# A linear-attention and expert kernel: shorter load queue, small zero matmuls, tiles amid the turns

## The chip, the cores and the metric

The kernel runs on one core of a Trainium2 chip. The metric is the time of one execution on the device in microseconds (us): lower is better. TensorE (PE) multiplies, VectorE (DVE), ScalarE (ACT) and GpSimd (POOL) do elementwise work, SyncE (SP) issues the loads and stores, and 16 DMA engines carry them. The engines run side by side and wait for each other through semaphores.

## The reference

Three steps follow one another. First a decayed linear attention without softmax, then a mixture of four ReLU experts, then a feed-forward layer with the Mish function. Everything is float32.

```
# q, k, v: 2 batches, 8 heads, 576 positions, 64 per head
scores = q @ k^T / sqrt(64)
x = (scores * gamma_h ** (i - j) for j <= i, else 0) @ v      # -> 1152 tokens x 512
p = domain_probs / (domain_probs.sum(-1) + 1e-9)              # 1152 x 4
y = sum over e of p[:, e] * (relu(x @ w1[e]) @ w2[e])         # w1: 4 x 512 x 1024
out = mish(y @ w_in) @ w_out                                  # 512 -> 2048 -> 512
```

## The kernel before

**Attention.** The 576 positions are cut into nine places of 64. Place c (the prediction calls its data pair c) needs two loads of 512 KB: `feats` (k and q by features) and `toks` (v and k by tokens). Four buffers (`SLOTS`) hold them, so place c shares a buffer with place c - 4. The loop over turns runs c = 0 to 8 on PE. In turn c PE first does `scores_and_state(c)`: the scores of place c + 1 (L442) and the update of the running state with place c (L447), interleaved; then `output(c)`: `of_state` (L470), which applies the state before place c, and `of_chunk` (L474), which applies the masked scores of place c. Each `pe.matmul` of float32 shows as two records with two weight loads, so `scores_and_state` is 64 records, and each half of `output` is 32.

The other engines serve this loop, each in a written order: POOL's `v_decay(c + 2)` (L1024) decays v of a place once its `toks` has landed; DVE's `masked(c)` (L812) masks the scores, `decayed(c - 1)` (L829) takes the output out of PSUM, `first_lo` (L836) and ACT's `first_hi` (L692) split it into a high and a low part; ACT's `state_copy(c)` (L686) copies the state for the next place. `rows(i)` (L818) makes tables of decay on DVE.

**Tiles amid the attention.** The first 384 of the 1152 tokens are complete after turn 2 (place 0, 1, 2). With them PE can start the first layer of expert 0: a tile is 12 matmuls of 384 columns (`plain_products`, L494 to L496, the three products of high and low parts). `TILES_IN` lists which of the eight tiles follow `output(c)` in which turn. Each tile needs its weights split: ACT's `job_hi` (L368), then POOL's `job_lo` (L395), listed by turn in `JOBS_IN`. In each turn POOL does `v_decay(c + 2)` first and then the jobs of the turn. `plain_ready` waits for the low part of the tile's weights and for the low parts of x (`s_xl`).

**Loads.** SP issues everything in one written order: the first load, `toks` 0, `feats` and `toks` of places 1 to 3 one after the other, then for each place from 4 on two weight loads of 256 KB (`WEIGHTS_IN`), a wait for `output(c - 4)` to free the buffer, and the pair; then the identity matrix and all other weights.

**Zero matmuls.** `keep_warm` multiplies zeros into bank 7: seven times 512 columns before the first load has landed, and five times after the scores of place 0.

**Behind the attention.** PE does `second(0, ...)`, 12 groups of three matmuls of 512 columns, and then stage 2, where one level of Strassen's scheme is used for the other 768 tokens: its products P1 and P2 use x directly (P1 of stage 2 waits for all nine `first_lo`), P6, P7, P5 and P4 use differences of blocks of x, made by DVE (L959 to L964), split by ACT's `t_hi` (L736) and DVE's `t_lo` (L918). P6 also waits for ACT's copy of P1 (`keep`, L722), which stands on ACT behind the `t_hi` and two weight jobs.

Of the kernel before, what the change touches and what calls it, by code (L numbers as in the profile page):

```python
# [13 lines left out]
P = 128  # L14
# [5 lines left out]
CH = 64  # L20
PLACES = SEQ // CH
PAIRS = HEADS // 2
MID = SEQ // 2
SLOTS = 4
# [8 lines left out]
KT = DM // P  # L33
# [13 lines left out]
def has_state(c):  # L47
# [5 lines left out]
STATE_BANK, OUT_BANK = 2, 3  # L53


TILES_IN = {3: (0,), 4: (1,), 5: (2, 3), 6: (4,), 7: (5, 6), 8: (7,)}
JOBS_IN = {1: (("w1", 0, 0),), 2: (("w1", 0, 1), ("w1", 0, 2)), 3: (("w1", 0, 3),), 4: (("w1", 0, 4), ("w1", 0, 5)),
           5: (("w1", 0, 6),), 6: (("w1", 0, 7), ("w2", 0, 0)), 7: (("w2", 0, 1), ("w2", 0, 2), ("s", 0, 0)),
           8: (("w2", 0, 3), ("w2", 0, 4)), 9: (("w2", 0, 5),)}

WEIGHTS_IN = (2, 2, 2, 2, 2)
ROWS_IN = {4: 5, 5: 6, 6: 7, 7: 8}
PROBS_IN = 5
WARM_START, WARM_NEXT = 7, 5

# [3 lines left out]
ITEMS = 4  # L71
# [98 lines left out]
def build(nc, first_in, feats_in, toks_in, ident_in, probs_in, weights_in, out):  # L170
    with ExitStack() as ctx:
# [125 lines left out]
        def landed(c):  # L297
            return 16 * (c // SLOTS + 1)
# [101 lines left out]
        @block.sync  # L400
        def _(sp):
            def load_feats(c):
                sp.dma_start(slots[:, c % SLOTS, 0:2], feats_in[c - 1]).then_inc(s_feats[c % SLOTS], 16)

            def load_toks(c):
                sp.dma_start(slots[:, c % SLOTS, 2:4], toks_in[c]).then_inc(s_toks[c % SLOTS], 16)

            def load_weights(r):
                job, e, layer, u = LOADS[r]
                if r >= RAW:  # L410
                    sp.wait_ge(s_wl, LOADS[r - RAW][0] + 1)
                sp.dma_start(w_raw[:, r % RAW], weights_in[2 * UNITS * e + UNITS * layer + u])\
                  .then_inc(s_raw[r % RAW], 16)

            sp.dma_start(loaded[:, lead - CONSTS:lead + 2 * KIND], first_in).then_inc(s_feats[0], 16)
            load_toks(0)
            for c in range(1, SLOTS):
                load_feats(c)
                load_toks(c)
            at = 0  # L420
            for c in range(SLOTS, PLACES):
                for r in range(at, at + WEIGHTS_IN[c - SLOTS]):
                    load_weights(r)
                at += WEIGHTS_IN[c - SLOTS]
                sp.wait_ge(s_o, c - SLOTS + 1)
                load_feats(c)
                load_toks(c)
            sp.dma_start(ident[:, :], ident_in).then_inc(s_id, 16)
            for r in range(at, len(LOADS)):
                load_weights(r)  # L430
            by_rows = out.rearrange("(g p) d -> p g d", p=P)
            sp.wait_ge(s_af, read(EXPERTS - 1, TT - 1))
            sp.dma_start(by_rows[:, 0:TT, :], acc_sb[:, 0:TT, :]).then_inc(s_out, 16)
            for g in range(TT, TPP):
                sp.wait_ge(s_af, read(EXPERTS - 1, g))
                sp.dma_start(by_rows[:, g, :], acc_sb[:, g, :]).then_inc(s_out, 16)
            sp.wait_ge(s_out, 16 * (1 + TPP - TT))

        @block.tensor
        def _(pe):  # L440
# [73 lines left out]
            def plain_products(s, i, tiles):  # L514
# [6 lines left out]
                if KT - 1 in tiles:  # L521
                    mm.then_inc(s_l1, 1)

            def product(s, j):

                e, g = s // STAGES, s % STAGES - 2
                n = sums(s)
                if j == P1:
                    if g == 0 and e >= MOE_EXPERTS:
                        pe.wait_ge(s_mi, mish_done(s - 1, 2))  # L530
                    elif g == 0:
                        pe.wait_ge(s_hl, ITEMS * (s - 1) + 3)
                    else:
                        pe.wait_ge(s_cc, ITEMS * (n - 1) + C21 + 1)
                    if s == 2:
                        pe.wait_ge(s_xl, PLACES)
                    if s == MOE_STAGES + 2:
                        pe.wait_ge(s_x2l, SPLIT_AT[2, KT - 1])
                if j == P2:
                    if g == 0 and e >= MOE_EXPERTS:  # L540
                        pe.wait_ge(s_mi, mish_done(s - 1, 3))
                    elif g == 0:
                        pe.wait_ge(s_hl, ITEMS * (s - 1) + 4)
                    else:
                        pe.wait_ge(s_cc, ITEMS * (n - 1) + C12 + 1)
                if j == P6:
                    pe.wait_ge(s_wl, JOB["s", e, g] + 1)
                if j in (P6, P7, P4):
                    pe.wait_ge(s_pt, 3 * n + (P6, P7, P4).index(j) + 1)
                if j in (P5, P3):  # L550
                    pe.wait_ge(s_cc, ITEMS * n + (C11 if j == P5 else C22) + 1)
                if e % MOE_EXPERTS == 0 and g == 0 and X_OF[j][0] == "t":
                    pe.wait_ge(s_tl, 4 * (e > 0) + T_ORDER.index(X_OF[j][1]) + 1)
                for k in range(KH):
                    at = slice(P * k, P * (k + 1))
                    if WEIGHTS_OF[j][0] == "w":
                        row, half = WEIGHTS_OF[j][1:]
                        cs = slice(P * (KH * half + k), P * (KH * half + k + 1))
                        w = w_hi[0][:, 2 * g + row, cs], w_lo[0][:, 2 * g + row, cs]
                    else:  # L560
                        w = w_sum(g)[:, 0, WEIGHTS_OF[j][1], at], w_sum(g)[:, 1, WEIGHTS_OF[j][1], at]
                    i = KH * X_OF[j][1] + k
                    x = (xb_hi[:, i], xb_lo[:, i]) if X_OF[j][0] == "x" else (xt[:, 0, i], xt[:, 1, i])
                    mm = three(banks[BANK_OF[j]][:, 0:TC], w, x, j in OPENS and k == 0, k == KH - 1,
                               skip_group_check=True)
                mm.then_inc(s_l1, 1)
# [49 lines left out]
            def keep_warm(count):  # L616

                for _ in range(count):
                    pe.matmul(banks[7][:, :], zeros[:, 0:P], zeros[:, :], start=True, stop=True)

            pe.wait_ge(s_zt, 1)
            keep_warm(WARM_START)
            pe.wait_ge(s_feats[0], landed(0))
            for h in range(HEADS):
                score(0, 0, h)
                mm = score(0, 1, h)
            mm.then_inc(s_sc, 1)
            keep_warm(WARM_NEXT)
            for c in range(PLACES):
                if has_state(c):  # L630
                    scores_and_state(c)
                output(c)
                for t in TILES_IN.get(c, ()):
                    s, i = divmod(t, ITEMS)
                    plain_ready(s, i)
                    plain_products(s, i, range(KT))

            for q in range(ITEMS * TT):
                second(0, q)
# [38 lines left out]
        def _(act):  # L678
# [53 lines left out]
            def t_hi(e, n):  # L732

                i = T_ORDER[n]
                act.wait_ge(s_tf, (9, 8, 6, 10)[n] if e else (3, 2, 1, 4)[n])
                act.activation(x_sum(i, 0), x_full(e, i), ACT.Copy).then_inc(s_th, 1)  # L736

            for c in range(TURNS):
                if c > 0:
                    first_hi(c - 1)  # L740
                for t in TILES_IN.get(c - 1, ()):
                    plain_hi(*divmod(t, ITEMS))
                if has_state(c):
                    state_copy(c)
                if c == PROBS_IN:
# [5 lines left out]
                for job in IN_TURN.get(c, ()):  # L751
                    if JOBS[job][0] != "s":
                        job_hi(act, job)
            for n in range(4):
                t_hi(0, n)
            for job in IN_STAGE[1]:
                job_hi(act, job)

            for s in range(2, ALL_STAGES):
                e, k = divmod(s, STAGES)  # L760
# [47 lines left out]
        def _(dve):  # L808
# [126 lines left out]
            for c in range(TURNS):  # L935
                if c < PLACES:
                    masked(c)
                if c == 0:
                    for i in range(2, 5):
                        rows(i)  # L940
                if c > 0:
                    decayed(c - 1)
                if c > 1 and c != PER_BLOCK + 1:
                    first_lo(c - 2)
                if c == PER_BLOCK:
                    first_lo(c - 1)
                for t in TILES_IN.get(c - 1, ()):
                    plain_lo(*divmod(t, ITEMS))
                if c in ROWS_IN:
                    rows(ROWS_IN[c])  # L950
                if c == PROBS_IN + 1:
                    probs()
            first_lo(PLACES - 1)


            b11, b21 = xf[:, 0:KH, 0:TC], xf[:, KH:, 0:TC]
            b12, b22 = xf[:, 0:KH, TC:], xf[:, KH:, TC:]
            full = [x_full(0, i) for i in range(4)]
            dve.tensor_tensor(full[0], b12, b11, ALU.subtract).then_inc(s_tf, 1)  # L959
            dve.tensor_tensor(full[2], b22, b12, ALU.subtract).then_inc(s_tf, 1)  # L960
            dve.wait_ge(s_tf, 1)
            dve.tensor_tensor(full[1], b22, full[0], ALU.subtract).then_inc(s_tf, 1)  # L962
            dve.wait_ge(s_tf, 3)
            dve.tensor_tensor(full[3], full[1], b21, ALU.subtract).then_inc(s_tf, 1)  # L964
            dve.wait_ge(s_tf, 4)
            for n in range(4):
                t_lo(0, n)

            for s in range(2, ALL_STAGES):
# [120 lines left out]
```

## Time and profile before

| | before |
|---|---|
| median of three runs | 621.67 us (620.61 to 621.79) |
| the profiled execution's own time | 622.52 us |
| its span | 620.7 us |
| PE busy in the span | 605.9 us, 98% |
| DVE, ACT, POOL busy | 264.0, 234.7, 278.2 us |
| moved by DMA | 50.47 MB |
| mean granted PE clock | 0.989 |

The span is the stretch between the first and the last instruction that the profiler shows; the execution's own time has 1.8 us more around it. Busy time of PE is that of its matmuls, whose ends are modelled. The granted clock is told as a share of full speed: 1.00 is 2.4 GHz, 0.50 is 1.2 GHz. In the lists of waits an idle stretch is put down to what ended it; "issue" means that the profile shows nothing that the engine waited for.

### The profile page before, as it was taken

What the parts mean: (1) busy time and instruction counts of PE and PEld (TensorE: products, weight loads), DVE (VectorE), ACT (ScalarE), POOL (GpSimd) and SP (SyncE); (2) the same over time, 40 slices, a digit from 0 to 9 for tenths busy, and PEclk for the clock granted to TensorE, in tenths of its full rate; (3) what the DMA queues carried; (4) which work ended last, traced back from release to release, by engine and by line L of the source; (5) the groups of instructions that cost most, each with busy time, mean ns of one, the idle gap of its engine ahead of it and who ended that gap; (6) DMA issues with size and microseconds to landing.
All of it is one profiled execution on the core that took longest, in us unless ns stands there. A gap on an engine that the chain in (4) does not pass through costs nothing.

```text
span 620.7 us, 9829 instructions
## 1 busy us (share of the span) xinstructions
PE 605.9 (98%) x4016; PEld 547.0 (88%) x4016; DVE 264.0 (43%) x361; ACT 234.7 (38%) x434; POOL 278.2 (45%) x230
## 2 busy tenths in 40 slices
PE   6799999999999999999999999999999999999997
PEld 4699799999999999999999999989989999989996
DVE  2467654423154434154534154535545432324334
ACT  2464433322323332223432123435455454334431
POOL 2658645535335544435552535532446553443300
PEclk9699999999999999999999999999999999999999
DMA  8963202332112331112322112321211232201002
GB/s 345 331 213 109 80 35 68 104 101 68 35 35 68 103 103 57 46 35 68 102 84 62 58 34 69 102 69 37 67 34 49 69 105 84 68 1 52 1 1 101
DMA packets 24923, 50.47 MB, mean 81 GB/s; under 512 B 2864, under 2 KB 2992, under 8 KB 24880
## 3 DMA queue, kind: packets, MB, share of 16 engines
q1 hardware_dynamic: 24736, 49.84, 25.1%
q8 instruction: 32, 0.52, 0.3%
q14 instruction: 11, 0.09, 0.1%
q10 hardware_dynamic: 144, 0.02, 0.0%
HBM read 47.49 MB, written 2.36 MB: 80 GB/s over the span
## 4 chain that ended last, share of the span: by engine, by line
PE 92%; DVE 2%; ACT 2%; issue 1%; DMA 1%; POOL 1%; SPq 0%
PE bank L494 30%; PE bank L496 29%; PE bank L495 29%; PE bank L442 1%; DMA loaded<-in_feats 1%; PE bank L470 1%; PE bank L612 1%; PE bank L474 1%; ACT xt L736 0%; ACT w_hi L368 0%; DVE acc_sb L888 0%; DVE acc_sb L892 0%; POOL w_lo L395 0%; DVE xs_a L962 0%; DVE xs_a L959 0%
## 5 line engine op out<-in xcount | busy, mean ns | idle before, releaser
L395 POOL TENSOR_TENSOR w_lo<-w_raw,w_hi 128x512 fp32r<-128x512 f32 x96 | 134.6, 1416 | 149.8 <-ACT w_hi L368 149.8
L494 PE MATMUL bank<-w_hi,h_hi 128*128 128x512 f32 x432 | 168.7, 391 | 0.0
L496 PE MATMUL bank<-w_hi,h_lo 128*128 128x512 f32 x432 | 168.3, 390 | 0.0
L495 PE MATMUL bank<-w_lo,h_hi 128*128 128x512 f32 x432 | 168.3, 390 | 0.0
L875 DVE TENSOR_TENSOR h_act<-part,bank 128x384 f32<-128x384 f32 x96 | 52.9, 551 | 169.9 <-PE bank L496 169.4
L390 POOL TENSOR_TENSOR ws<-ws_f,ws 128x1024 fp32r<-128x1024 f32 x24 | 57.6, 2401 | 145.1 <-ACT ws L364 145.1
L496 PEld LDWEIGHTS bank<-w_hi,h_lo 128*128 128x128 f32 x432 | 81.1, 188 | 16.9
L495 PEld LDWEIGHTS bank<-w_lo,h_hi 128*128 128x128 f32 x432 | 81.1, 188 | 12.3
L494 PEld LDWEIGHTS bank<-w_hi,h_hi 128*128 128x128 f32 x432 | 81.0, 188 | 12.1
L722 ACT ACTIVATE part<-bank 128x384 f32<-128x384 f32 x72 | 35.3, 491 | 138.6 <-PE bank L496 138.6
L842 DVE SCALAR_TENSOR_TENSOR h_lo<-h_act,h_hi 128x384 fp32r<-128x384 f32 x64 | 73.2, 1153 | 20.5 <-ACT h_hi L712 19.9
L494 PE MATMUL bank<-xa_hi,w_hi 128*128 128x384 f32 x192 | 66.2, 345 | 0.0
L496 PE MATMUL bank<-xa_hi,w_lo 128*128 128x384 f32 x192 | 65.2, 339 | 0.0
L495 PE MATMUL bank<-xa_lo,w_hi 128*128 128x384 f32 x192 | 65.1, 339 | 0.0
L849 DVE TENSOR_TENSOR h_lo<-h_act,h_hi 128x384 fp32r<-128x384 f32 x48 | 38.2, 796 | 55.5 <-ACT h_hi L717 55.1
L368 ACT ACTIVATE w_hi<-w_raw 128x512 fp32r<-128x512 f32 x96 | 57.0, 619 | 4.2 <-DMA w_raw<-in_weights 4.0
L712 ACT ACTIVATE h_hi<-h_act 128x384 fp32r<-128x384 f32 x64 | 33.5, 525 | 59.9 <-DVE h_act L875 59.8
L494 PE MATMUL bank<-xt,ws 128*128 128x384 f32 x144 | 48.6, 337 | 1.3 <-issue 1.1
L842 DVE SCALAR_TENSOR_TENSOR h_lo<-bank,h_hi 128x384 fp32r<-128x384 f32 x32 | 17.8, 556 | 72.3 <-ACT h_hi L703 72.3
L496 PE MATMUL bank<-xt,ws 128*128 128x384 f32 x144 | 48.4, 336 | 0.0
L495 PE MATMUL bank<-xt,ws 128*128 128x384 f32 x144 | 48.4, 336 | 0.0
L703 ACT ACTIVATE h_hi<-bank 128x384 fp32r<-128x384 f32 x32 | 15.7, 491 | 76.6 <-PE bank L496 76.6
(88 smaller groups left out, 863.0 us busy)
## 6 DMA issues: line engine op xcount, KB each, us to landing
w_raw<-in_weights SPq DMA_DIRECT2D x144, 256.0 KB, 2.7
loaded<-in_toks SPq DMA_DIRECT2D x9, 512.0 KB, 7.0
loaded<-in_feats SPq DMA_DIRECT2D x8, 512.0 KB, 6.2
out<-acc_sb SPq DMA_DIRECT2D x6, 256.0 KB, 2.1
out<-acc_sb SPq DMA_DIRECT2D x1, 768.0 KB, 3.5
loaded<-in_first SPq DMA_DIRECT2D x1, 726.0 KB, 4.4
ident<-in_ident SPq DMA_DIRECT2D x1, 64.0 KB, 5.0
p_nat<-in_probs ACTq DMA_DIRECT2D x1, 18.0 KB, 5.1
```

The source lines that it names most:

```text
L368: act.activation(w_hi[int(kind == "w2")][:, x], w_raw[:, r % RAW], ACT.Copy).then_inc(s_wh, 1)
L390: pool.tensor_tensor(w_sum(x)[:, 1], ws_f[:, :], w_sum(x)[:, 0].bitcast(F32), ALU.subtract)\
L395: pool.tensor_tensor(w_lo[layer][:, x], w_raw[:, r % RAW], w_hi[layer][:, x].bitcast(F32), ALU.subtract).then_inc(s_wl, 1)
L494: pe.matmul(out, w[0], x[0], start=first, stop=False, **more)
L495: pe.matmul(out, w[0], x[1], start=False, stop=False, **more)
L496: return pe.matmul(out, w[1], x[0], start=False, stop=last, **more)
L703: act.activation(h_hi[:, tile_slot(s, i)], banks[6 + i % 2][:, 0:TC], ACT.Relu).then_inc(s_hh, 1)
L712: act.activation(h_hi[:, tile_slot(s, i)], h_act[:, i % 2], ACT.Relu).then_inc(s_hh, 1)
L722: act.activation(part[:, i], banks[6][:, 0:TC], ACT.Copy).then_inc(s_pt, 1)
L842: dve.scalar_tensor_tensor(h_lo[:, slot], full, 0.0, h_hi[:, slot].bitcast(F32), ALU.max, ALU.subtract).then_inc(s_hl, 1)
L849: dve.tensor_tensor(h_lo[:, slot], h_act[:, i % 2], h_hi[:, slot].bitcast(F32), ALU.subtract)\
L875: dve.tensor_tensor(h_act[:, i % 2], part[:, kept], banks[bank][:, 0:TC], op).then_inc(s_cc, 1)
```

## The change

The zero matmuls become 72 of 64 columns ahead of the first load, in one quarter of the array, and those after the scores of place 0 go. Five tiles move between `scores_and_state` and `output` of their turn (`TILE_AMID`), three stay after `output` (`TILE_AFTER`); DVE and ACT take them up in the matching order. The weight jobs of turn 1 move to turn 2. From place 2 on SP issues `feats` of a place only when `feats` of the place before has landed, and `toks` when `toks` before has landed; from place 4 on the two weights go out after the wait for `feats`, and the pair after the wait for `toks`. The decay tables are made earlier. Behind the last turn DVE makes the differences of x ahead of, and between, the last low parts, and ACT does its two weight jobs ahead of `t_hi`.

```diff
-TILES_IN = {3: (0,), 4: (1,), 5: (2, 3), 6: (4,), 7: (5, 6), 8: (7,)}
-JOBS_IN = {1: (("w1", 0, 0),), 2: (("w1", 0, 1), ("w1", 0, 2)), 3: (("w1", 0, 3),), 4: (("w1", 0, 4), ("w1", 0, 5)),
-           5: (("w1", 0, 6),), 6: (("w1", 0, 7), ("w2", 0, 0)), 7: (("w2", 0, 1), ("w2", 0, 2), ("s", 0, 0)),
+TILE_AMID = {3: 0, 4: 1, 5: 2, 6: 4, 7: 5}
+TILE_AFTER = {5: 3, 7: 6, 8: 7}
+JOBS_IN = {2: (("w1", 0, 0), ("w1", 0, 1)), 3: (("w1", 0, 2),), 4: (("w1", 0, 3), ("w1", 0, 4)),
+           5: (("w1", 0, 5), ("w1", 0, 6)), 6: (("w1", 0, 7), ("w2", 0, 0)),
...
-ROWS_IN = {4: 5, 5: 6, 6: 7, 7: 8}
+ROWS_IN = {0: (2, 3), 1: (4, 5), 2: (6,), 3: (7, 8)}
-WARM_START, WARM_NEXT = 7, 5
+WARM = 72
...
             load_toks(0)
-            for c in range(1, SLOTS):
+            load_feats(1)
+            load_toks(1)
+            for c in range(2, SLOTS):
+                sp.wait_ge(s_feats[(c - 1) % SLOTS], landed(c - 1))
                 load_feats(c)
+                sp.wait_ge(s_toks[(c - 1) % SLOTS], landed(c - 1))
                 load_toks(c)
             at = 0
             for c in range(SLOTS, PLACES):
+                sp.wait_ge(s_feats[(c - 1) % SLOTS], landed(c - 1))
                 for r in range(at, at + WEIGHTS_IN[c - SLOTS]):
                     load_weights(r)
                 at += WEIGHTS_IN[c - SLOTS]
                 sp.wait_ge(s_o, c - SLOTS + 1)
+                sp.wait_ge(s_toks[(c - 1) % SLOTS], landed(c - 1))
                 load_feats(c)
                 load_toks(c)
...
-                    pe.matmul(banks[7][:, :], zeros[:, 0:P], zeros[:, :], start=True, stop=True)
+                    pe.matmul(banks[7][HALF[0], 0:CH], zeros[:, 0:CH], zeros[:, 0:CH], start=True, stop=True)
...
                 if has_state(c):
                     scores_and_state(c)
+                if c in TILE_AMID:
+                    early_tile(TILE_AMID[c])
                 output(c)
-                for t in TILES_IN.get(c, ()):
-                    s, i = divmod(t, ITEMS)
-                    plain_ready(s, i)
-                    plain_products(s, i, range(KT))
+                if c in TILE_AFTER:
+                    early_tile(TILE_AFTER[c])
...
+            for job in IN_STAGE[1]:
+                job_hi(act, job)
             for n in range(4):
                 t_hi(0, n)
-            for job in IN_STAGE[1]:
-                job_hi(act, job)
...
-            first_lo(PLACES - 1)
...
+            dve.wait_ge(s_xt, PLACES)
             dve.tensor_tensor(full[0], b12, b11, ALU.subtract).then_inc(s_tf, 1)
-            dve.tensor_tensor(full[2], b22, b12, ALU.subtract).then_inc(s_tf, 1)
             dve.wait_ge(s_tf, 1)
             dve.tensor_tensor(full[1], b22, full[0], ALU.subtract).then_inc(s_tf, 1)
-            dve.wait_ge(s_tf, 3)
+            plain_lo(*divmod(TILE_AFTER[PLACES - 1], ITEMS))
+            dve.tensor_tensor(full[2], b22, b12, ALU.subtract).then_inc(s_tf, 1)
+            t_lo(0, 0)
+            first_lo(PLACES - 1)
+            dve.wait_ge(s_tf, 2)
             dve.tensor_tensor(full[3], full[1], b21, ALU.subtract).then_inc(s_tf, 1)
-            dve.wait_ge(s_tf, 4)
-            for n in range(4):
+            for n in range(1, 4):
                 t_lo(0, n)
```

## Rows read from the trace of the kernel before

**Rows 1.** The page: busy us of each engine, share of the span and instructions.
```profile
PE 605.9 (98%) x4016; PEld 547.0 (88%) x4016; DVE 264.0 (43%) x361; ACT 234.7 (38%) x434; POOL 278.2 (45%) x230
```

**Rows 2.** Windows: length, busy us (records) of each engine, PE clock, DMA share, GB/s.
```profile
0.00:31.06 31.06, 20.96 (x536) 16.63 (x536) 11.35 (x16) 10.95 (x17) 13.28 (x16) 0.79 0.91 338
31.06:55.97 24.91, 24.91 (x661) 23.57 (x661) 17.27 (x29) 14.96 (x27) 15.15 (x13) 0.99 0.53 176
55.97:76.00 20.03, 18.71 (x88) 15.83 (x88) 14.15 (x13) 8.83 (x17) 14.50 (x10) 1.00 0.32 93
```

**Rows 3.** Waits of PE, first 31.4 us: total us, times, longest.
```profile
PE bank L470 <- issue: 6.7, 3, 2.7
```

**Rows 4.** Timeline of PE: start, us, line, operation [idle before <- what ended it].
```profile
1.31 3.08 PE L619 MATMUL bank<-zeros 128*128 128x512 bf16 x7 [1.31 <-POOL zeros L1019]
...
5.17 1.15 PE L442 MATMUL bank<-loaded 64*64 64x64 f32 x32 [0.78 <-DMA loaded<-in_first]
...
7.77 0.27 PE L442 MATMUL bank<-loaded 64*64 64x64 f32 x2 [0.26 <-DMA loaded<-in_feats]
...
10.47 0.27 PE L442 MATMUL bank<-loaded 64*64 64x64 f32 x2 [1.07 <-DMA loaded<-in_feats]
...
17.09 0.64 PE L470 MATMUL bank<-loaded,st 64*64 64x64 f32 x14
...
20.48 0.46 PE L470 MATMUL bank<-loaded,st 64*64 64x64 f32 x17 [2.74 <-issue]
...
26.93 0.69 PE L494 MATMUL bank<-xa_hi,w_hi 128*128 128x384 f32 x1
...
31.06 0.37 PE L442 MATMUL bank<-loaded 64*64 64x64 f32 x2
...
46.29 0.27 PE L442 MATMUL bank<-loaded 64*64 64x64 f32 x2
...
69.56 0.41 PE L494 MATMUL bank<-xt,ws 128*128 128x384 f32 x1 [1.12 <-issue]
```

**Rows 5.** Windows between the stops of PE.
```profile
7.77:11.90 4.13, 3.06 (x177) 2.78 (x177) 2.26 (x6) 1.99 (x4) 1.20 (x2) 1.00 1.03 417
14.20:17.74 3.54, 3.54 (x126) 3.35 (x127) 1.77 (x3) 1.48 (x3) 1.91 (x2) 0.53 1.03 403
20.48:23.60 3.12, 3.12 (x127) 2.93 (x126) 2.05 (x3) 1.20 (x3) 2.79 (x4) 0.62 0.91 297
```

**Rows 6.** DMA queues from 17.9 to 18.1 us: packets, MB, share of 16 engines.
```profile
q8 instruction: 1, 0.02, 33.8%
```

**Rows 7.** Timeline of POOL.
```profile
9.14 1.04 POOL L1024 TENSOR_TENSOR loaded<-loaded 128x512 f32<-128x512 f32 x1 [1.59 <-DMA loaded<-in_toks]
...
25.20 1.28 POOL L395 TENSOR_TENSOR w_lo<-w_raw,w_hi 128x512 fp32r<-128x512 f32 x1 [0.75 <-ACT w_hi L368]
```

**Rows 8.** Single loads, by line: issue length and start, then issue to landing.
```profile
L403 SPq DMA_DIRECT2D loaded<-in_feats x1: 328/328/328, 33.4 to 33.4; - x1
...
DMA to landing us min/median/max: 3.8/3.8/3.8
...
L406 SPq DMA_DIRECT2D loaded<-in_toks x1: 433/433/433, 33.8 to 33.8; - x1
...
DMA to landing us min/median/max: 5.3/5.3/5.3
...
L406 SPq DMA_DIRECT2D loaded<-in_toks x1: 1167/1167/1167, 27.4 to 27.4; - x1
...
DMA to landing us min/median/max: 6.7/6.7/6.7
```

**Rows 9.** Timelines of DVE (two rows) and ACT ahead of stage 2.
```profile
62.92 2.04 DVE L962 TENSOR_TENSOR xs_a<-xf,xs_a 128x768 f32<-128x768 f32 x1
...
66.35 0.96 DVE L918 TENSOR_TENSOR xt<-xs_a,xt 128x768 fp32r<-128x768 f32 x1 [0.40 <-DVE xs_b L964]
...
68.99 0.47 ACT L722 ACTIVATE part<-bank 128x384 f32<-128x384 f32 x1
```

More of the change, by code:

```diff
@@ L53 @@
 STATE_BANK, OUT_BANK = 2, 3
-TILES_IN = {3: (0,), 4: (1,), 5: (2, 3), 6: (4,), 7: (5, 6), 8: (7,)}
-JOBS_IN = {1: (("w1", 0, 0),), 2: (("w1", 0, 1), ("w1", 0, 2)), 3: (("w1", 0, 3),), 4: (("w1", 0, 4), ("w1", 0, 5)),
-           5: (("w1", 0, 6),), 6: (("w1", 0, 7), ("w2", 0, 0)), 7: (("w2", 0, 1), ("w2", 0, 2), ("s", 0, 0)),
-           8: (("w2", 0, 3), ("w2", 0, 4)), 9: (("w2", 0, 5),)}
+TILE_AMID = {3: 0, 4: 1, 5: 2, 6: 4, 7: 5}
+TILE_AFTER = {5: 3, 7: 6, 8: 7}
+JOBS_IN = {2: (("w1", 0, 0), ("w1", 0, 1)), 3: (("w1", 0, 2),), 4: (("w1", 0, 3), ("w1", 0, 4)),
+           5: (("w1", 0, 5), ("w1", 0, 6)), 6: (("w1", 0, 7), ("w2", 0, 0)),
+           7: (("w2", 0, 1), ("w2", 0, 2), ("s", 0, 0)), 8: (("w2", 0, 3), ("w2", 0, 4)), 9: (("w2", 0, 5),)}
 WEIGHTS_IN = (2, 2, 2, 2, 2)
-ROWS_IN = {4: 5, 5: 6, 6: 7, 7: 8}
+ROWS_IN = {0: (2, 3), 1: (4, 5), 2: (6,), 3: (7, 8)}
 PROBS_IN = 5
-WARM_START, WARM_NEXT = 7, 5
+WARM = 72
 STAGES = 6
@@ L522, in plain_products, with early_tile @@
                     mm.then_inc(s_l1, 1)
+            def early_tile(t):
+                s, i = divmod(t, ITEMS)
+                plain_ready(s, i)
+                plain_products(s, i, range(KT))
             def product(s, j):
@@ L618, in keep_warm @@
                 for _ in range(count):
-                    pe.matmul(banks[7][:, :], zeros[:, 0:P], zeros[:, :], start=True, stop=True)
+                    pe.matmul(banks[7][HALF[0], 0:CH], zeros[:, 0:CH], zeros[:, 0:CH], start=True, stop=True)
             pe.wait_ge(s_zt, 1)
-            keep_warm(WARM_START)
+            keep_warm(WARM)
             pe.wait_ge(s_feats[0], landed(0))
@@ L627, in _ @@
             mm.then_inc(s_sc, 1)
-            keep_warm(WARM_NEXT)
             for c in range(PLACES):
@@ L734, in t_hi @@
                 i = T_ORDER[n]
-                act.wait_ge(s_tf, (9, 8, 6, 10)[n] if e else (3, 2, 1, 4)[n])
+                act.wait_ge(s_tf, (9, 8, 6, 10)[n] if e else (2, 3, 1, 4)[n])
                 act.activation(x_sum(i, 0), x_full(e, i), ACT.Copy).then_inc(s_th, 1)
@@ L740, in _ @@
                     first_hi(c - 1)
-                for t in TILES_IN.get(c - 1, ()):
-                    plain_hi(*divmod(t, ITEMS))
+                if c - 1 in TILE_AFTER:
+                    plain_hi(*divmod(TILE_AFTER[c - 1], ITEMS))
                 if has_state(c):
@@ L753, in _ @@
                         job_hi(act, job)
+                if c in TILE_AMID:
+                    plain_hi(*divmod(TILE_AMID[c], ITEMS))
+            for job in IN_STAGE[1]:
+                job_hi(act, job)
             for n in range(4):
                 t_hi(0, n)
-            for job in IN_STAGE[1]:
-                job_hi(act, job)
             for s in range(2, ALL_STAGES):
@@ L937, in _ @@
                     masked(c)
-                if c == 0:
-                    for i in range(2, 5):
-                        rows(i)
                 if c > 0:
@@ L946, in _ @@
                     first_lo(c - 1)
[L947 to L950, printed above, removed]
+                for i in ROWS_IN.get(c, ()):
+                    rows(i)
+                if c - 1 in TILE_AFTER and c < PLACES:
+                    plain_lo(*divmod(TILE_AFTER[c - 1], ITEMS))
                 if c == PROBS_IN + 1:
                     probs()
-            first_lo(PLACES - 1)
+                if c in TILE_AMID:
+                    plain_lo(*divmod(TILE_AMID[c], ITEMS))
             b11, b21 = xf[:, 0:KH, 0:TC], xf[:, KH:, 0:TC]
```

## The prediction

> **What bounds the kernel now.** I read the page first. TensorE (PE) is busy 98% of the span [rows 1], so whatever can be won lies where it isn't busy, or where its clock is low. The windows say where that is [rows 2]: in the first 31.06 us PE has 20.96 us of work and a mean clock of 0.79; from there to 55.97 it is busy throughout, at full clock; to 76 it misses 1.3 us of 20; the whole page's 605.9 us of PE leaves little for the rest: 620.7 less 605.9 is 14.8 us of pauses, and 10.1 + 0 + 1.3 of them lie ahead of 76. So only the attention stage and the entry to stage 2 can give anything.
>
> The chain of waits for PE names three waits of "issue", 6.7 us together, all at L470, of_state [rows 3]. No wait stands inside that group of matmuls in the code: not half of its 32 records have run, PE stops, and the last 17 run 2.74 us later [rows 4]. Between one stop and the next PE runs 126 or 127 matmul records and as many weight loads, and the stretches with stops between them show it [rows 5]. One packet of the instruction queue, 0.02 MB (the page has 32 packets for 0.52 MB, so 16 KB each), begins at 17.9 us, just after the stop of 17.74, and PE goes on 2.6 us later [rows 6]. I read the stops as PE out of instructions: a block holds some 127 matmuls with their loads, a turn without a tile is 128 records, and the block after next is fetched by the same 16 DMA engines that carry the loads at 400 GB/s. A block costs 14.20 to 20.48, 6.28 us, in the fullest queue and 20.48 to 25.24, 4.76 us, in the next, against 3.1 to 3.5 us of matmuls in it [rows 5]. Where a tile of 12 long matmuls is in the block there is no stop.
>
> The Trainium skill ("Runtime: NRT & Kernel Launch", Instruction fetch mechanics) gives blocks of 16 KiB and 256 instructions, and says that the cost of a block's edge is mostly hidden. The size agrees with the packet; the hiding doesn't, at 6.7 us. By that rule the stops would have another cause and the shorter queue would give nothing; that is weighed as the third rival.
>
> The second loss is the clock: 0.53 and 0.62 in two of the running stretches [rows 5], so that tile 0 begins at 26.93 and turn 4 at 31.06 [rows 4], 4.13 us for a tile that takes some 2.1 at full clock.
>
> **Zero matmuls.** 12 of 512 columns go, 72 of 64 columns come. The seven at the start take 3.08 us from 1.31 to 4.39 [rows 4], 440 ns each; an eighth of the columns is 55 ns, 72 of them 4.0 us, to 5.3, where scores of pair 0 begin at 5.17. If each also shows its weight load, twice that at most, so 1.31 + 7.9 = 9.2 with no rise of the clock, near 7 with one. Pair 1 isn't in before 7.77, so 0 to 1.5 us are late at turn 0, and behind it turn 1 waits for pair 2 anyway (below). I take 0. The main effect is the shift: 60 more records come ahead. The first stop fell on record 17 of of_state in turn 1, 81 into the turn; it moves to record 21 of turn 1, where PE has just waited for pair 2. The next edges come in the scores of turns 2 and 3.
>
> **Loads.** First, toks 0, feats 1 and toks 1 go as before; toks 1 lands at 9.14, when GpSimd (POOL) takes it [rows 7]. Then feats 2 waits for feats 1 (7.8), toks 2 for toks 1, and so on. What a load costs in a short queue is shown by the last pairs: feats 8, issued at 33.4, 3.8 us; toks 8, issued 0.4 later, 5.3; toks 7, issued at 27.4, 6.7 [rows 8]. For one load alone I take 3.6 (3.0 to 3.8: part of the 3.8 is the remainder of the loads ahead). feats 2: 11.4; feats 3: 15.0; toks 2: 12.7; toks 3: 16.3. So turn 1 begins 0.9 us later than at 10.47 [rows 4], and turn 2 at 15.0. From pair 4 on feats and toks are issued together once toks of the pair before are in, and two weights a little ahead of them. One round is then 5.7 us by pair 8 (33.4 to 39.1), 7.1 by pair 7 (27.0 to 34.1), and 4.8 if feats take 3.6 and toks follow at the 400 GB/s seen before. For pair 4, with only 1.5 MB in flight, I take 5.2: toks 4 in at 21.5. Queued on SP behind each wait are this pair and all weights after it; those beyond the first ten start about when toks 7 is in, 37 to 39 instead of 35.5, and ScalarE (ACT) wants the first of them in turn 7, past 45.
>
> **Instruction blocks against that.** Edges at 11.7, then 4.8 to 6.3 later each: 16.5 to 18.0, and 21.3 to 24.3. The 45 records of scores behind the last edge take 0.7 to 1.3. So turn 3 has its scores done at 22 to 25.5; I take 22.5. The 6.7 us of stops shrink to about 3, but the scores of turn 3 aren't much earlier than the third run's 20.48 to 23.60: the loads take their place.
>
> **Tile 0 ahead of the output.** It needs the low part of weight 0. That job moves from turn 1 to turn 2, and on POOL stands behind the decay of v for pair 4, thus behind toks 4. 21.5 + 1.04 for the decay, 1.28 for the subtraction [rows 7], and 0.1: tile 0 starts at 24.0 (earliest 23.0, latest 26 with a round of 7.1), instead of 26.93. Its 4.13 us at half clock, then the output, which the old order had ahead of it: 1.7 at half and 0.95 at full clock; turn 4 begins at 24.0 + 4.13 + 1.4 = 29.5 instead of 31.06, 1.5 us sooner. Before, the clock rose 6.2 us after unbroken work began at 25.24; now that begins at 24.0, so the rise comes at 30.2 or sooner, worth up to 0.4: 1.9 in all. From there PE has the same work as in the 24.91 us to 55.97, and at a round of 5.2 to 5.7 each pair is in before its turn (feats 8 by 41.5, turn 7 at 44.4: 46.29 [rows 4] less 1.9). The 1.9 stays.
>
> **Entry to stage 2.** PE pauses 1.12 us ahead of 69.56 because ACT's copy of `part` ends at 69.5 [rows 4, 9]; ACT waited for VectorE's (DVE) third difference at 62.92 (2.04 us while POOL works, 0.96 for as many elements when it doesn't) and then did two weight jobs, 1.1 us. Now the differences start when the last pair is decayed, some 3 us sooner, and the jobs come first. I take the pause and the 0.2 after it as gone: 1.1 (low 0.3: `first_lo(8)`, which PE needs for its first product, now stands behind three differences and a `t_lo`, 8 us at 2.04 each, just the length of the 12 `second` groups ahead of it; high 1.4). The moved `rows` cost nothing: DVE is busy 11.35 of 31.06 us [rows 2].
>
> **Sum.** 1.9 + 1.1 = 3.0 us. The profiled execution took 622.52, 620.7 of it span, so 619.5; it lies 0.85 over the median of the three runs, 621.67, which gives 618.7.
>
> **Rivals.**
> 1. Full clock from tile 0 on: the first 72 matmuls and denser turns keep it at 2.4 GHz. Tile 0 and the output then take 2.1 + 0.95 instead of 5.5: 2.5 us more, 1.9 + 2.5 + 1.1 = 5.5, 616.2, and with tile 0 at 23.2 another 0.8. For it: a full clock at 7.77 to 11.90 [rows 5]. Against it: PE still waits near 9.4, 13, 15 and 22 us. 0.18.
> 2. Only the start gives: the differences on DVE meet POOL and stage 2 waits as long as before. 621.67 - 1.9 = 619.8. 0.14.
> 3. The stops aren't cured by a shorter queue or only change place: 6.3 us per block and a late toks 4 put tile 0 at 26, and 0.3 + 0.3 us remain: 621.1, no change. 0.13.
> 4. Slower: a round takes 7.1 us, as pair 7 showed. toks 4 lands at 23.4, toks 7 at 44.7, feats 8 at 49, and turn 7, which began at 46.29, waits for it: 2.7 later, less 1.1 at stage 2: 623.3. It decides from a round of 6.8 on. For it: the one pair issued into a nearly empty queue took that long. The Trainium skill ("DMA: Bandwidth & Descriptors", Rules for kernel authors) speaks for it too: issue a load early and wait late, since the fixed cost then overlaps. Against it: pair 8 took 5.7. 0.13.
>
> **Numbers.** Forecast 0.42, rivals 0.18, 0.14, 0.13, 0.13. Faster by over 0.2% (1.24 us, about what a measurement of this kernel can tell from no change): 0.42 + 0.18 + 0.14 = 0.74; within it 0.13; slower 0.13. The range 615.5 to 622.0 leaves out rival 4 and a little of rival 1; the forecast's own is 617.0 to 620.0.
>
> **What the profile will show.** Tile 0 (L494 with xa_hi) starting at 23 to 25, turn 4 by 29.5; SP waiting on landings; feats 2 at some 11.4 and rounds of 5 to 6 us; PE's issue waits down to about 3 us; the busy stretch from tile 0 to the first `second` as long as before; no pause ahead of the first product from `xt`. Wrong if the clock rises before tile 0, if rounds pass 6.8 us, or if PE still stops as often inside turns.

## The result and the profile after

The change makes the kernel slower: 628.35 us median of four runs (627.54 to 630.24) against 621.68, a ratio of 1.0112 (95% interval 1.0098 to 1.0126). I had forecast 618.7, range 615.5 to 622.0. The profiled execution took 628.2 us, 626.4 of it span, 5.7 more than the span of before. In one experiment below, the change with large zeros, two of four runs had a mean granted clock of 0.65 and 0.75 and took 866.21 and 759.82 us; its figures are those of the other two.

| stretch | before | after | difference |
|---|---|---|---|
| to the start of turn 4 | 31.06 | 32.80 | +1.74 |
| turns 4 to 8, to the first `second` | 24.91 | 28.61 | +3.70 |
| from there to P7 of stage 2 | 16.48 | 16.72 | +0.24 |
| sum | | | +5.68 |

The starts of before are in [rows 2] and [rows 4]; P7 began at 72.45. Behind P7 the two spans are alike: the three rows of the table hold all of the 5.7 us.

The waits of PE after the change (engine, line, what it waited for: total us, times, longest):

```profile
PE bank L449 <- DMA loaded<-in_feats: 9.0, 4, 5.2
PE bank L481 <- issue: 2.5, 2, 1.4
```

The 6.7 us of "issue" at `of_state` [rows 3] are gone, as the loads were thinned out. In their place PE waits 9.0 us for `feats`, and 2.5 us of "issue" now stand at L481, `of_chunk`, and later. The timeline of PE, changed kernel:

```profile
1.31 3.92 PE L632 MATMUL bank<-zeros 128*64 128x64 bf16 x72 [1.31 <-POOL zeros L1034]
...
11.73 0.37 PE L449 MATMUL bank<-loaded 64*64 64x64 f32 x2 [0.81 <-DMA loaded<-in_feats]
...
23.77 0.37 PE L449 MATMUL bank<-loaded 64*64 64x64 f32 x2 [5.23 <-DMA loaded<-in_feats]
...
27.35 0.69 PE L501 MATMUL bank<-xa_hi,w_hi 128*128 128x384 f32 x1 [1.59 <-POOL w_lo L396]
...
32.80 0.22 PE L449 MATMUL bank<-loaded 64*64 64x64 f32 x1
...
38.62 0.34 PE L481 MATMUL bank<-loaded 64*64 64x64 f32 x8 [1.43 <-issue]
...
44.22 0.57 PE L481 MATMUL bank<-loaded 64*64 64x64 f32 x22 [1.06 <-issue]
...
51.39 0.22 PE L449 MATMUL bank<-loaded 64*64 64x64 f32 x1
...
61.41 0.39 PE L501 MATMUL bank<-w_hi,h_hi 128*128 128x512 f32 x1
...
78.13 0.45 PE L501 MATMUL bank<-xt,ws 128*128 128x384 f32 x1 [1.82 <-ACT part L734]
```

The row at 1.31 is all 72 zero matmuls: 3.92 us. Its 128*64 says that they use half of the array, not a quarter. Pair 2 comes at 11.73, pair 4 only at 23.77, behind a wait of 5.23 us. Tile 0 waits for POOL until 27.35, where I had 24.0 and before had 26.93 [rows 4], and runs at half clock (0.50 from 27.35 to 31.49). Turn 4 starts at 32.80. Then PE stops twice more, at 38.62 and 44.22, inside output, where before there was no stop inside the turns behind 25.24; turns 7 and 8 without a stop take 10.02 us (51.39 to 61.41) against 9.68 before (46.29 to 55.97).

Three windows of the changed kernel (columns as in [rows 2]): from 10 to 20 us, turns 4 to 8, and from the end of one late stop to the end of the next.

```profile
10.00:20.00 10.00, 6.65 (x292) 6.19 (x284) 6.35 (x11) 4.82 (x8) 2.68 (x3) 0.74 0.84 257
32.80:61.41 28.61, 26.12 (x673) 23.86 (x666) 17.17 (x27) 14.82 (x28) 17.76 (x16) 1.00 0.72 235
38.62:44.22 5.60, 4.54 (x127) 4.07 (x127) 2.79 (x4) 3.35 (x6) 3.52 (x3) 1.00 0.88 278
```

257 GB/s at a DMA share of 0.84; the kernel before moved 404 at 1.03 from 10 to 20 us. In turns 4 to 8 PE is busy for 26.12 of 28.61 us: 2.49 is the two stops. Between them it runs 127 matmul records, tile 2 among them: the same block length as in [rows 5], so a tile in the block doesn't keep the stop away. The other 1.21 us of the 3.70 are 0.14 in turn 4, 0.68 in turn 5, 0.05 in turn 6 and 0.34 in turns 7 and 8 (turns' lengths less the stops, against before).

SP's queue, `feats` of pairs 4 to 8 in the changed kernel (start and length of the issue):

```profile
18.27 0.33 SPq L404 DMA_DIRECT2D loaded<-in_feats  x1
...
25.03 1.03 SPq L404 DMA_DIRECT2D loaded<-in_feats  x1
...
31.04 0.33 SPq L404 DMA_DIRECT2D loaded<-in_feats  x1
...
38.11 0.33 SPq L404 DMA_DIRECT2D loaded<-in_feats  x1
...
44.90 0.33 SPq L404 DMA_DIRECT2D loaded<-in_feats  x1
```

Each goes out when `toks` of the pair before has landed, so their distances are the rounds: 6.8, 6.0, 7.1 and 6.8 us. I had taken 5.2 to 5.7. By then more than two loads are queued: two weight loads of 256 KB go out ahead of each pair. For pair 4, `feats` and `toks` by themselves:

```profile
L404 SPq DMA_DIRECT2D loaded<-in_feats x1: 327/327/327, 18.3 to 18.3; - x1
...
DMA to landing us min/median/max: 5.5/5.5/5.5
...
L407 SPq DMA_DIRECT2D loaded<-in_toks x1: 433/433/433, 18.6 to 18.6; - x1
...
DMA to landing us min/median/max: 6.3/6.3/6.3
```

5.5 and 6.3 us from issue to landing. The loads ahead of them, which I had put at 3.6 us each, took 3.5 (`feats` 2), 4.5 (`toks` 2), 4.7 (`feats` 3) and 4.2 (`toks` 3), so that pair 4 went out at 18.27, where the prediction's times have 16.3. POOL then shows the chain that I described: `toks` 4 taken at 25.04 (3.5 us late), the decay, and the low parts of weights 0 and 1.

```profile
25.04 1.04 POOL L1039 TENSOR_TENSOR loaded<-loaded 128x512 f32<-128x512 f32 x1 [5.74 <-DMA loaded<-in_toks]
...
26.04 2.51 POOL L396 TENSOR_TENSOR w_lo<-w_raw,w_hi 128x512 fp32r<-128x512 f32 x2
```

### The profile page after: what moved, and what is told of

Same layout as the page of the kernel before. It is cut to its first block, busy times and chain, and to the rows that moved or that the text cites. A ratio compares the mean times of both kernels' runs of the same rounds, so it can differ in the third digit from the quotient of the medians.

```text
span 626.4 us, 9954 instructions
## 1 busy us (share of the span) xinstructions
PE 606.8 (97%) x4076; PEld 550.3 (88%) x4076; DVE 264.5 (42%) x361; ACT 234.8 (37%) x434; POOL 279.7 (45%) x230
## 4 chain that ended last, share of the span: by engine, by line
PE 89%; DMA 3%; DVE 3%; ACT 2%; POOL 1%; issue 1%; SPq 0%; DVEq 0%
PE bank L501 29%; PE bank L503 29%; PE bank L502 29%; DMA loaded<-in_feats 2%; DVE xt L932 1%; DMA loaded<-in_toks 1%; ACT w_hi L369 1%; PE bank L625 1%; PE bank L449 1%; POOL w_lo L396 0%; PE bank L477 0%; PE bank L481 0%; ACT st L698 0%; DVE acc_sb L902 0%; DVE acc_sb L906 0%
## 5 line engine op out<-in xcount | busy, mean ns | idle before, releaser
L889 DVE TENSOR_TENSOR h_act<-part,bank 128x384 f32<-128x384 f32 x96 | 53.0, 552 | 170.7 <-PE bank L503 170.2
```

What stands on the lines that cost most here:

```text
L889: dve.tensor_tensor(h_act[:, i % 2], part[:, kept], banks[bank][:, 0:TC], op).then_inc(s_cc, 1)
```

## The experiments

Ratios are to the kernel before, with 95% intervals, from runs on the same chip; its medians there were 621.75 to 622.0 us.

| run | median us | ratio | interval |
|---|---|---|---|
| change, loads issued as before | 624.37 | 1.0041 | 1.0020 to 1.0063 |
| before, waits on landings alone | 629.24 | 1.0120 | 1.0103 to 1.0138 |
| change, waits for places 2 and 3 only | 625.93 | 1.0064 | 1.0041 to 1.0088 |
| before, 72 small zeros alone | 627.23 | 1.0084 | 1.0063 to 1.0104 |
| before, new entry to stage 2 alone | 622.25 | 1.0000 | 0.9988 to 1.0011 |
| before, five tiles amid alone | 624.65 | 1.0043 | 1.0029 to 1.0056 |
| before, four loads in flight | 622.62 | 1.0007 | 0.9994 to 1.0020 |
| change, large zeros (two runs) | 630.11 | 1.0128 | 1.0099 to 1.0158 |
| before, tile 0 alone amid | 623.93 | 1.0032 | 1.0019 to 1.0046 |
| before, three loads in flight | 624.24 | 1.0035 | 1.0012 to 1.0058 |
| before, entry with early sum | 620.25 | 0.9971 | 0.9959 to 0.9983 |
| before, tile 0 amid and entry with early sum | 621.87 | 1.0003 | 0.9988 to 1.0018 |
| before, 139 small zeros | 624.64 | 1.0046 | 1.0031 to 1.0062 |
| before, entry with early sum, old order of ACT | 620.48 | 0.9975 | 0.9964 to 0.9986 |

**The waits on landings.** First out of the change, then alone on the kernel before, then for the first places only.

```diff
 e1: the changed kernel, SP
-                sp.wait_ge(s_feats[(c - 1) % SLOTS], landed(c - 1))
-                sp.wait_ge(s_toks[(c - 1) % SLOTS], landed(c - 1))
 e2: the kernel before, SP: the same waits added as in the change, nothing else
 e3: the changed kernel, in the loop over places 4 to 8 only
-                sp.wait_ge(s_feats[(c - 1) % SLOTS], landed(c - 1))
-                sp.wait_ge(s_toks[(c - 1) % SLOTS], landed(c - 1))
```

> The changed kernel with the loads issued as before (no wait for a landing). Theory A: the loss is the rounds of 6 to 7 us that the waits on landings make; feats 4 landed at 23.75 and stopped PE for 5.2 us, and stops inside output came later for the same reason. Then this kernel loses them and takes 617 to 621 us, at or below the kernel before. Theory B: the loss is the tiles amid the turns and the weight jobs of turn 1 moved behind the decay of place 4; then tile 0 still starts at 26 or later, and the time stays at 625 to 628.

> The kernel before with the waits on landings alone. Theory A: 625 to 629 us, with PE waiting some 5 us for feats 4. Theory B: at most 1 us from the 621.7 of before, since the three stops of 6.7 us go where the loads' waits come.

> The changed kernel with the waits on landings for places 2 and 3 only; from place 4 on the loads go out as before. Theory A, if the rounds from place 4 on are what costs: feats 4 is issued at about 14.4 instead of 18.3 and lands by 20, tile 0 starts near 24, and the time is 620 to 623. If the waits of places 2 and 3 already cost, 624 or more. Theory B: 625 to 628.

The waits alone cost 7.2 us (629.24 against 622.0), by themselves as much as the whole change. Taking them out of the change brings back 4.0 (628.35 to 624.37), but not the time of before: theory A had 617 to 621, so something else in the change costs too. In its trace that lies behind turn 4, which begins at 30.03 (before: 31.06): from there to the first `second` at 56.97 it takes 26.94 us against 24.91. With the waits for places 2 and 3 only, 625.93 us, above the 623 of theory A with free first waits. That is 1.6 over the version without any wait, but the two intervals overlap, so that the first waits cost too is likely and not shown. The timeline of PE with the waits alone:

```profile
17.84 0.46 PE L476 MATMUL bank<-loaded,st 64*64 64x64 f32 x17 [0.46 <-issue]
...
23.04 0.37 PE L448 MATMUL bank<-loaded 64*64 64x64 f32 x2 [4.27 <-DMA loaded<-in_feats]
...
29.35 0.66 PE L500 MATMUL bank<-xa_hi,w_hi 128*128 128x384 f32 x1 [2.62 <-DVE xa_lo L842]
```

The stop at `of_state` in turn 2 shrinks from 2.74 [rows 4] to 0.46 us, and the four stops of "issue" in this trace are 3.2 us in all. But two of them (1.07 us at 40.71, 1.39 at 52.53) stand in turns 5 and 7, where before had none, `feats` 4 stops PE for 4.27 us, and tile 0 starts at 29.35.

**How many loads in flight.**

```diff
 e7: the kernel before, four in flight (a load waits for the one two places before)
-            for c in range(1, SLOTS):
+            load_feats(1), load_toks(1), load_feats(2), load_toks(2)
+            for c in range(3, SLOTS):
+                sp.wait_ge(s_feats[(c - 2) % SLOTS], landed(c - 2))
                 load_feats(c)
+                sp.wait_ge(s_toks[(c - 2) % SLOTS], landed(c - 2))
                 load_toks(c)
...
 e10: three in flight (toks(c) waits for feats(c - 1), feats(c + 1) for toks(c - 1))
```

> The kernel before with waits on landings as changed, but one place later: a load goes out when the one two places before has landed, so four loads are in flight instead of two. Theory A1: the long rounds come from too few loads in flight (257 GB/s at a DMA share of 0.8 against 404 at 1.03); then four in flight give at least 350 GB/s from 10 to 20 us, place 4 lands by 20.5, and the time is 621 to 624. Theory A2: any wait for a landing costs, whatever its depth: 627 to 629.

> The kernel before with three loads in flight instead of two (before: all; two: 629.2 us; four: 622.6). If the time follows the rate at which loads land: about 300 GB/s from 10 to 20 us, place 4 in at 20 to 22, stops of 1 to 2 us in place of 2.3 to 2.7, and 622 to 625. If a shorter queue buys shorter stops without a price at this depth: 619 to 621.

From 10 to 20 us, four loads in flight:

```profile
10.00:20.00 10.00, 6.09 (x283) 5.75 (x276) 3.56 (x6) 4.49 (x8) 3.80 (x5) 0.83 1.00 366
```

| in flight | GB/s, 10 to 20 us | DMA share | time us |
|---|---|---|---|
| two (alone) | 245 | 0.80 | 629.24 |
| three | 309 | 0.93 | 624.24 |
| four | 366 | 1.00 | 622.62 |
| all (before) | 404 | 1.03 | 621.75 to 622.0 |

The time follows the rate. It isn't the wait as such that costs (A2 falls), it is that two loads of 512 KB don't fill the engines. Nor did any depth gain: with four the stops for instructions are 6.9 us in all, as long as before, and with three 8.3, longer than before. So a shorter queue did not by itself shorten the stops; only with two in flight, at 245 GB/s, were they short.

**The zero matmuls.**

```diff
 e4 and e14: the kernel before
-WARM_START, WARM_NEXT = 7, 5
+WARM = 72                     (e14: 139)
-                    pe.matmul(banks[7][:, :], zeros[:, 0:P], zeros[:, :], start=True, stop=True)
+                    pe.matmul(banks[7][HALF[0], 0:CH], zeros[:, 0:CH], zeros[:, 0:CH], start=True, stop=True)
-            keep_warm(WARM_NEXT)
 e8: the changed kernel with those lines as before
```

> The kernel before with the 72 small zero matmuls in place of the 12 large ones. My reading of instruction blocks: 60 more matmul records ahead move each stop by 60 records earlier, from of_state of turns 1, 2, 3 into the scores of the same turns; the stops stay about as long, 5 to 7 us in all, and the time stays within 1.5 us of 621.7. If the stops have another cause, tied to of_state, they stay at L470.

> The changed kernel with the 12 large zero matmuls of before in place of the 72 small ones. Those alone cost 5.2 us on the kernel before, since the edges of the instruction blocks moved. If they cost as much in the changed kernel: 623 to 624. If the waits for loads cover the stops there: 627 to 629.

> The kernel before with 139 small zero matmuls in place of the 12 large ones: 127 more records, as many as one instruction block holds, against 60 more in the run with 72. If the place of the block edges in the turns is what cost 5.2 us there, the edges fall where they fell before: three stops at of_state in turns 1 to 3 and none in turns 4 to 6, and 621.5 to 624 us, the 139 matmuls themselves ending near 8 us, 1 to 2 us late for turn 0 and mostly hidden. If it is their number, or the missing large ones after the scores of place 0, it stays at 627 or more.

The 72 alone cost 5.2 us where I had 0. The stops, in the timeline of PE with them:

```profile
18.02 0.37 PE L447 MATMUL bank<-loaded 64*64 64x64 f32 x2 [3.31 <-issue]
...
24.30 0.26 PE L442 MATMUL bank<-loaded 64*64 64x64 f32 x1 [2.46 <-issue]
...
29.54 0.33 PE L442 MATMUL bank<-loaded 64*64 64x64 f32 x4
...
35.77 0.44 PE L495 MATMUL bank<-xa_lo,w_hi 128*128 128x384 f32 x1 [2.56 <-issue]
...
41.88 0.39 PE L474 MATMUL bank<-loaded 64*64 64x64 f32 x10 [1.04 <-issue]
...
60.57 0.39 PE L494 MATMUL bank<-w_hi,h_hi 128*128 128x512 f32 x1
```

From the end of the stop at 35.77 to the end of the next (columns as in [rows 2]):

```profile
35.77:41.88 6.11, 5.07 (x127) 4.57 (x128) 1.58 (x3) 2.30 (x4) 1.71 (x3) 0.72 0.70 250
```

The stops did move from `of_state` to the scores (3.31 and 2.46 us, turns 2 and 3), 60 records ahead, as the block reading says. But two new ones came behind 31 us, 2.56 inside a tile and 1.04 inside output, and the granted clock fell to a mean of 0.66 from 36 to 41 us; the first `second` starts at 60.57 instead of 55.97. Turn 4 starts at 29.54, 1.5 us sooner than before, and from there to the first `second` it takes 31.03 us instead of 24.91: the whole loss lies behind the start of turn 4. Between the two new stops there are 127 matmul records again. The pages count the same blocks: 32 packets of the instruction queue for 8032 records of PE before (4016 matmuls and as many weight loads), 33 for 8286 with 139 zeros, 251 to a packet in both. With 139, the edges are back:

```profile
12.14 0.37 PE L447 MATMUL bank<-loaded 64*64 64x64 f32 x2 [2.90 <-issue]
...
22.87 0.69 PE L470 MATMUL bank<-loaded,st 64*64 64x64 f32 x14 [2.76 <-issue]
...
26.95 0.80 PE L470 MATMUL bank<-loaded,st 64*64 64x64 f32 x17 [0.39 <-issue]
...
32.48 0.27 PE L442 MATMUL bank<-loaded 64*64 64x64 f32 x2
...
57.18 0.39 PE L494 MATMUL bank<-w_hi,h_hi 128*128 128x512 f32 x1
```

Stops are at `of_state` again (2.76 and 0.39 in the rows above, 0.38 in turn 1), none behind 27 us, and turn 4 to the first `second` takes 24.70 us (32.48 to 57.18) as before's 24.91. One new stop of 2.90 us in turn 0 is paid for the extra block, and the time is 624.64. So what the 72 cost behind turn 4 is the place of the edges there, and not the size of the matmuls. In the changed kernel taking the 72 out gained nothing (ratio 1.0128); that the waits for loads cover the edges there fits, and no trace shows it. Why the edges in turns 4 and 5 stop PE in one position and not in another isn't read off any row; that a block with fewer tile matmuls in it is run through sooner than the next one is fetched fits, and wasn't measured by itself.

**The tiles amid the turns.**

```diff
 e6: the change without its zeros, its waits and its entry to stage 2
 e9: the kernel before
-TILES_IN = {3: (0,), 4: (1,), ...
+TILES_IN = {4: (1,), ...
+                if c == 3:
+                    plain_ready(0, 0)
+                    plain_products(0, 0, range(KT))
                 output(c)
 (and plain_hi(0, 0), plain_lo(0, 0) at the end of turn 3)
```

> The kernel before with the tiles amid the turns, the weight jobs and the decay tables moved, and nothing else: large zeros, deep load queue, old entry to stage 2. By the block reading: no block of 127 records without a tile from turn 3 on in either order, so the stops stay at three in turns 1 to 3 and the time depends on tile 0, which waits for the decay of place 4 (19.4 + 1.0 + 1.3, so before 22) and for the split of places 1 and 2: within 2 us of before, likelier faster (619 to 622). If the order amid the turns is itself bad: 624 or more.

> The kernel before with tile 0 alone moved between the scores and the output of turn 3; all other tiles, jobs, zeros and loads as before. With all five tiles amid, turn 4 began 1.9 us sooner than before (29.14 against 31.06), and it was given back: 1.1 us of stops for instructions in turns 5 and 6, the rest in more changes between tiles and turns. If that is so, tile 0 alone keeps most of it: 619.5 to 621.5. If the stops come wherever the turns run sooner, because the fetches wait behind the same loads: 621.5 to 623.

Tile 0, turn 4 and the first `second` with all five amid, from the timeline of PE:

```profile
23.86 0.66 PE L495 MATMUL bank<-xa_hi,w_hi 128*128 128x384 f32 x1 [0.78 <-DVE xa_lo L845]
...
29.14 0.22 PE L443 MATMUL bank<-loaded 64*64 64x64 f32 x1
...
55.73 0.39 PE L495 MATMUL bank<-w_hi,h_hi 128*128 128x512 f32 x1
```

Tile 0 starts at 23.86 and turn 4 at 29.14: 1.92 us sooner than before, as I had worked out (24.0 and 29.5). But the first `second` starts at 55.73, only 0.24 sooner, and P7 at 72.68, 0.23 later than before. Over all its runs the kernel is 0.4% slower; the traced run, 622.75 us, is the fastest of the eight, so where the median's 2.9 us go isn't seen. Tile 0 alone amid is slower as well, 0.3%: my expectation that it keeps the gain fell. There tile 0 starts at 26.00 and runs at a clock of 0.50, and turn 4 starts at 31.30, no sooner than before.

**The entry to stage 2.**

```diff
 e5: the kernel before with the change's orders of DVE and ACT behind the last turn
 e12: e5, and on DVE
-            for n in range(1, 4):
+            t_lo(0, 1)
+            add_parts(2, C11)
+            for n in range(2, 4):
                 t_lo(0, n)
...
 e15: e12 with ACT's two weight jobs behind t_hi as before
 e13: e12 and e9 together
```

> The kernel before with the new entry to stage 2 alone (differences of x earlier on VectorE, ScalarE's two weight jobs ahead of t_hi). My prediction had 1.1 us gained. What the changed kernel showed: the product P7 began 16.72 us after the first second group against 16.48 before, since VectorE's last t_lo ends as late (15.2 us after it, each t_lo 2.04 us beside GpSimd) and P7 waits for the chain behind it. By that this kernel takes 0 to 0.5 us more than before; if the gain was real and only hidden, 620.5.

> The kernel before with the new entry to stage 2 and, besides, VectorE's first sum of stage 2 (C11) moved ahead of the last two t_lo. Theory: P7 waited 1.66 us for ScalarE's copy of P6, which stands behind the split of C11, which stands behind VectorE's sum, which stood behind all four t_lo. Then the wait goes and the time is 620.0 to 621.0, 1.0 to 1.7 under the entry alone. If P7 or P5 then waits for the last t_lo instead: 621.5 to 622.5.

> Tile 0 alone amid turn 3 and the entry with the early sum together, on the kernel before. If both are gains and add: 618 to 620. If the first is none: as the entry with the early sum alone, 620 to 621.

> The entry with the early sum on the kernel before, with ScalarE's two weight jobs left behind its four t_hi as before. With the jobs first, GpSimd's two low parts run while VectorE makes differences, and each takes 2.04 us instead of 0.96. If that matters for P7 or P5, this is 0.3 to 1 us faster than the 620.25 us of the run with the jobs first; if PE waits for nothing there any more, the two are equal within 0.3 us.

The entry alone is no gain (1.0000). Why is in the changed kernel's own rows, of DVE and then of ACT:

```profile
71.24 2.05 DVE L932 TENSOR_TENSOR xt<-xs_b,xt 128x768 fp32r<-128x768 f32 x1
...
73.21 2.04 DVE L932 TENSOR_TENSOR xt<-xs_a,xt 128x768 fp32r<-128x768 f32 x1
...
75.18 1.50 DVE L932 TENSOR_TENSOR xt<-xs_b,xt 128x768 fp32r<-128x768 f32 x1
...
76.60 0.54 DVE L889 TENSOR_TENSOR h_act<-part,bank 128x384 f32<-128x384 f32 x1
```

```profile
77.18 0.52 ACT L724 ACTIVATE h_hi<-h_act 128x384 fp32r<-128x384 f32 x1 [4.60 <-DVE h_act L889]
...
77.61 0.47 ACT L734 ACTIVATE part<-bank 128x384 f32<-128x384 f32 x1
```

The three last `t_lo` (L932) take 2.05, 2.04 and 1.50 us and end at 76.7; then comes the sum for C11 (L889), then ACT's split of it (77.18), then ACT's copy of P6 (77.61), and P7 starts at 78.13. The differences started sooner, but the queue of DVE ended no sooner: the sum starts 15.19 us behind the first `second`, against 14.95 before (70.92 less 55.97). Before, three of the four `t_lo` took 0.95 to 0.96 us [rows 9]; now the last three take 1.50 to 2.05. P7 waits for the end of this queue. I had stopped at P6. With the sum ahead of the last two `t_lo`, first `second` and P7:

```profile
55.67 0.39 PE L494 MATMUL bank<-w_hi,h_hi 128*128 128x512 f32 x1
...
70.42 0.34 PE L494 MATMUL bank<-xt,ws 128*128 128x384 f32 x1
```

14.75 us from one to the other instead of 16.48, and PE (the first busy value) has no pause at all from 60 to 80 us:

```profile
60.00:80.00 20.00, 20.00 (x100) 17.92 (x99) 17.40 (x16) 6.79 (x11) 18.47 (x14) 1.00 0.39 119
```

That is 1.7 us, and the time is 620.25, ratio 0.9971: the one version that beats both kernels. ACT's order doesn't matter (0.9975). With tile 0 amid added, the gain is gone:

```profile
25.35 0.41 PE L494 MATMUL bank<-xa_hi,w_hi 128*128 128x384 f32 x1 [1.54 <-DVE xa_lo L841]
...
28.61 0.22 PE L442 MATMUL bank<-loaded 64*64 64x64 f32 x1
...
31.25 0.69 PE L470 MATMUL bank<-loaded,st 64*64 64x64 f32 x32 [1.51 <-issue]
...
38.27 0.27 PE L442 MATMUL bank<-loaded 64*64 64x64 f32 x1 [2.61 <-issue]
...
57.94 0.39 PE L494 MATMUL bank<-w_hi,h_hi 128*128 128x512 f32 x1
```

Turn 4 starts at 28.61, 1.7 us sooner than the 30.32 of the same kernel without the move, and then PE stops for 1.51 and 2.61 us, and the first `second` is at 57.94 instead of 55.67. The version with tile 0 alone amid is the same program up to there. It started turn 4 at 31.30, mostly because its tile 0 ran at a clock of 0.50 and not 1.00, had 1.3 us of stops behind it, and reached the first `second` at 58.01: turn 4 sooner by 2.7 us, the end of the stage by 0.07. From the end of its first late stop to the end of the second PE runs 128 matmul records (31.25 to 38.27), a block, and a packet of the instruction queue begins 2 to 3 us before PE goes on each time. I read it that the sooner turns met their instructions missing; these are single traces.

## Why the prediction was wrong

- **The loads, the step that failed.** "For one load alone I take 3.6" and "For pair 4, with only 1.5 MB in flight, I take 5.2". With two in flight the loads behind `feats` 2 took 4.2 to 4.7, then 5.5 for `feats` 4 and 6.3 for `toks` 4, and the four rounds from 18.27 to 44.90 took 6.7 us on average. `toks` 4 was in at 25.0 instead of 21.5. I had read a round of 7.1 in the trace (pair 7), and set it aside for 5.7 (pair 8), which had been issued with other loads in flight. The waits alone cost 7.2 us.
- **Rival 4 was right in cause and side, wrong in place and size.** It had `feats` 8 stop turn 7, 1.6 us over before. It was `feats` 4 that stopped PE, for 5.2 us, and nothing behind pair 4 did. The Trainium skill's rule that I named there ("DMA: Bandwidth & Descriptors", Rules for kernel authors: issue early and wait late, since the fixed cost then overlaps) agrees with this case: 245 GB/s and 629.24 us with two in flight, 404 and 622.0 with all issued ahead.
- **Zero matmuls: "I take 0."** They took 3.92 us, as worked out (4.0), and hid. What I had called their main effect, the shift of the edges, I followed only through turn 3. Alone it costs 5.2 us, in its trace all of it behind the start of turn 4.
- **Instruction blocks: right as far as they went.** The stops moved with 60 more records ahead, came back with 127 more, and shrank with two loads in flight, though not with three or four. "Where a tile of 12 long matmuls is in the block there is no stop" was a rule taken from one position of the edges, and it's false: 2.49 us of stops in turns 4 and 5 after, with tile 2 between them.
- **Tile 0 ahead of the output: right in mechanism.** It waited for `toks` 4, decay and low part, 3.3 us later than forecast, through the loads. All five tiles amid, with the loads and zeros of before, gave the 1.9 us at turn 4 in the traced run; tile 0 alone amid did not (31.30) in its own. The 0.4 of it that I gave to an earlier rise of the clock wasn't measured by itself: the clock during tile 0 was 0.50 in the changed kernel and with all five or tile 0 alone amid, and 1.00 with tile 0 amid and the early sum. "The 1.9 stays" failed: PE gave it back in the next turns.
- **Entry to stage 2: 1.1 us, measured 0 alone, and 0.24 lost in the changed kernel.** The pause ahead of P6 went; the one ahead of P7 grew from 0.20 to 1.82 us, since DVE's sum still stood behind all `t_lo`.
- **What the parts add up to.** Alone 7.2, 5.2 and 2.9 us (medians less that of before) and 0 for the entry (by its ratio), 15.3; together 6.7. They overlap; that waits for loads cover edges of blocks would do it, and is argued, not shown. How the 6.7 splits over the four can't be said, and why the 1.21 us of turns 4 to 8 that aren't stops arose stays open.

## What to carry to other kernels

When a trace shows PE stopping inside a group of matmuls without a wait, count the records between the stops and look for packets of the instruction queue: here 60 more small matmuls ahead moved the stops and made new ones some 30 us later, so follow the edges to the end of the stage. Before throttling loads, take the price of a load from the emptiest queue in the trace and keep the worst row that was really issued that way; here two loads of 512 KB in flight lost 39% of the rate (245 of 404 GB/s). When a producer is moved up, ask what stands last in its engine's queue, and move that: here moving one sum ahead gained what the reordering ahead of it hadn't.

## What the runs showed that I had not expected

- The rate at which these loads land grows with how many are in flight, well beyond two: 245, 309, 366 and 404 GB/s for two, three, four and all, with the DMA share at 0.80, 0.93, 1.00 and 1.03.
- Starting turn 4 sooner did not end the stage sooner: 28.61 to 57.94 and 31.30 to 58.01 with tile 0 amid turn 3, 30.32 to 55.67 without.
- PE stopped with few loads in flight too: in the changed kernel `toks` 6 went out at 31.41 and landed at 38.0, the packet of the instruction queue began between 36.4 and 36.5, and PE, stopped at 37.2, went on at 38.62. That the fetch waited behind `toks` 6 fits; no row shows when it was asked for.
